# Attention followed by two MLP layers: where the two halves of an attention output are added, and where the gpsimd queue takes v_lo

## The reference

```python
# attention, B, H, S, D = 2, 8, 768, 64
q_bits = (einsum('bhsd,dk->bhsk', q, proj) > 0)          # 6 bits; k_bits alike
mask   = q_bucket[:, :, :, None] == k_bucket[:, :, None, :]
scores = where(mask, q @ k.T / 8, -1e9)
attn   = softmax(scores);  o = attn @ v                   # per head
# x = o as (1536, 512), then
h = x @ w_in;  g = s * relu(h)**2 + b;  y = g @ w_out     # d_ff = 2048
out = ((y @ w1) * (y @ w2)) @ w3 @ w_out2                 # d_ff = 1024
```

## Time and profile before

| | |
|---|---|
| median of 3 runs | 803.09 us (801.74 to 803.3) |
| the profiled execution | 801.51 us |
| its span | 799.7 us |
| PE busy | 765.9 us (96%) |
| DVE busy | 459.5 us (57%) |
| ACT busy | 369.8 us (46%) |
| POOL busy | 239.0 us (30%) |
| attention part | 0 to about 287 us |

### The profile page before, as it was taken

How to read it: one execution, slowest core, us unless ns; L and a number is a source line. 1 busy time by engine, 2 the same in 40 slices (tenths; PEclk the granted TensorE clock), 3 DMA queues, 4 the chain that set the end, 5 groups by cost and what they waited for, 6 DMA issues and landing times.

```text
span 799.7 us, 11232 instructions
## 1 busy us (share of the span) xinstructions
PE 765.9 (96%) x3680; PEld 626.1 (78%) x3680; DVE 459.5 (57%) x809; ACT 369.8 (46%) x686; POOL 239.0 (30%) x150
## 2 busy tenths in 40 slices
PE   3999999999989989999999999999999999999998
PEld 2787787877878778888888888888887888888886
DVE  4898998998979921276565665656575201210220
ACT  2887898888979942353223232222342211211211
POOL 3346564565655564663021120210012000000000
PEclk9999999999999999999999999999999999999999
DMA  6343333433353222233010110101010000001001
GB/s 148 78 118 74 75 92 83 110 75 84 80 135 84 66 88 86 100 105 106 2 52 1 53 53 0 52 0 53 1 52 1 1 32 21 1 14 39 0 0 52
DMA packets 17680, 45.37 MB, mean 57 GB/s; under 512 B 4946, under 2 KB 6994, under 8 KB 17650
## 3 DMA queue, kind: packets, MB, share of 16 engines
q1 hardware_dynamic: 17650, 44.99, 20.4%
HBM read 37.75 MB, written 3.19 MB: 51 GB/s over the span
## 4 chain that ended last, share of the span: by engine, by line
PE 72%; POOL 9%; DMA 6%; ACT 5%; issue 3%; DVE 3%; SPq 1%; POOLq 0%; ACTq 0%
PE psum L987 54%; PE psum L1074 8%; DMA r_sb<-r_rows 4%; PE psum L941 3%; ACT prob L525 3%; PE psum L928 3%; POOL x_raw L389 2%; POOL raw L364 2%; POOL km L374 1%; PE psum L917 1%; ACT pt_hi L541 1%; PE psum L911 1%; POOL both_hi L369 1%; POOL vs L379 1%; DVE x_lo L864 1%
## 5 line engine op out<-in xcount | busy, mean ns | idle before, releaser
L760 DVE TENSOR_TENSOR pt_lo<-psum,pt_hi 128x384 fp32r<-128x384 f32 x192 | 97.8, 550 | 19.5 <-ACT pt_hi L541 18.1
L525 ACT ACTIVATE prob<-psum,exp_at 128x768 f32<-128x768 f32 x96 | 96.4, 1005 | 10.3 <-DVE exp_at L753 10.2
L541 ACT ACTIVATE pt_hi<-psum 128x384 fp32r<-128x384 f32 x192 | 84.2, 494 | 27.9 <-PE psum L928 26.7
L746 DVE TENSOR_REDUCE top<-psum 128x1 f32<-128x768 f32 x96 | 90.9, 946 | 4.2 <-PE psum L917 4.0
L633 ACT ACTIVATE relu<-psum 128x512 f32<-128x512 f32 x48 | 28.6, 597 | 137.2 <-PE psum L987 137.2
L987 PE MATMUL psum<-x_hi,w_b 128*128 128x512 f32 (+1 forms) x288 | 90.6, 396 | 0.0
L987 PE MATMUL psum<-x_hi,w_c 128*128 128x512 f32 (+1 forms) x288 | 90.5, 396 | 0.0
L928 PE MATMUL psum<-ident,prob 128*128 128x128 f32 x576 | 83.4, 280 | 4.4 <-DVE pt_lo L760 4.1
L887 DVE TENSOR_TENSOR ab<-psum,a_sb 128x512 f32<-128x512 f32 x24 | 16.6, 692 | 121.3 <-ACT a_sb L683 121.3
L841 DVE SCALAR_TENSOR_TENSOR relu<-psum,relu 128x512 f32<-128x512 f32 x48 | 33.1, 689 | 87.9 <-ACT relu L633 82.8
L403 POOL TENSOR_TENSOR w_b<-stage,w_b 128x1024 fp32r<-128x1024 f32 x18 | 43.7, 2427 | 126.5 <-ACT w_b L552 125.8
(11 more groups left out here) (91 smaller groups left out, 1481.5 us busy)
## 6 DMA issues: line engine op xcount, KB each, us to landing
raw<-in_qk SPq DMA_DIRECT2D x30, 384.0 KB, 5.2
stage<-in_w_out SPq DMA_DIRECT2D x12, 512.0 KB, 3.3
stage<-in_w3t SPq DMA_DIRECT2D x8, 512.0 KB, 3.8
stage<-in_w_in SPq DMA_DIRECT2D x8, 512.0 KB, 3.2
stage<-in_w SPq DMA_DIRECT2D x8, 512.0 KB, 3.2
raw_v<-in_v SPq DMA_DIRECT2D x16, 192.0 KB, 2.8
qm<-both_hi SPq DMA_DIRECT2D x16, 192.0 KB, 2.7
r_sb<-r_rows SPq DMA_DIRECT2D x16, 192.0 KB, 5.4
```

Of the source, the lines that this page charges most:

```text
L525: act.activation(prob[:, t % 3], score[t % 2], ACT.Exp, bias=exp_at[:, t % 2, 1:2], scale=exp_at[:, t % 2, 0:1], accum_out=rsum[:, (t // 6 ...
L541: act.activation(pt_hi[:, u % 2, 3 * part:3 * part + 3, (t % 3) * P:(t % 3 + 1) * P], turned[part].rearrange("p (j q) -> p j q", j=3), ACT ...
L746: dve.tensor_reduce(top[:, t % 2, 1:2], score[t % 2], AX.X, ALU.max, negate=True).then_inc(top_done, 1)
L760: dve.tensor_tensor(pt_lo[at], turned[part].rearrange("p (j q) -> p j q", j=3), pt_hi[at].bitcast(F32), ALU.subtract).then_inc(pt_lo_done, 1)
```

## The change

ACT copies both halves out of PSUM: the one that changes rows into `o_part`, which now has two buffers, and the other into `o_sum`. Both count `o_part_done`, and PE may overwrite bank 6 after both. POOL adds them, in place in `o_sum`, directly before the product in `x_of`; DVE's `o_add` is gone. ACT's copies wait for the product of the unit four before (`x_done`) instead of the DVE's add. Since that count is not positive in pair 1, ACT's loop starts at pair 2 and pair 1 is written out. On POOL both v_lo of a pair come ahead of the x_of of the same stretch, and in the last two pairs the weight remainders change places with x_of. The scratch area for dynamic DMAs is set to 1024 bytes; the kernel has no such DMA.

```diff
-            o_part = sb("o_part", [P, HALF], F32, a)
+            o_part = sb("o_part", [P, 2, HALF], F32, a)
...
             def x_of(u, unit, pr):
+                rows = slice(0, HD) if unit < 2 else slice(HD, P)
+                pool.wait_ge(o_part_done, 2 * u + 2)
+                pool.tensor_tensor(o_sum[rows, unit % 2], o_sum[rows, unit % 2], o_part[rows, unit % 2],
+                                   ALU.add).then_inc(o_sum_done, 1)
                 pool.wait_ge(o_sum_done, u + 1)
...
                 if not first:
+                    v_lo(2 * pr, 0)
+                    pool.wait_ge(v_lo_done, 2 * pr + 1)
                     x_of(4 * pr - 2, 2, pr - 1)
                     pool.wait_ge(x_done, 4 * pr - 1)
+                if before_last:
+                    w_out2_low(0)
                 if not last:
                     scale_q(pr + 1, 1)
                     pool.wait_ge(q_scaled, 2 * pr + 4)
                 if not first:
-                    v_lo(2 * pr, 0)
-                    pool.wait_ge(v_lo_done, 2 * pr + 1)
-                    if before_last:
-                        w_out2_low(0)
-                    if last:
-                        w_out2_low(2)
                     x_of(4 * pr - 1, 3, pr - 1)
                     pool.wait_ge(x_done, 4 * pr)
                 if last:
+                    w_out2_low(2)
                     w_out2_low(3)
...
+                v_lo(2 * pr + 1, 1)
+                pool.wait_ge(v_lo_done, 2 * pr + 2)
                 x_of(4 * pr, 0, pr)
                 pool.wait_ge(x_done, 4 * pr + 1)
-                v_lo(2 * pr + 1, 1)
-                pool.wait_ge(v_lo_done, 2 * pr + 2)
                 if before_last:
                     w_out2_low(1)
-                if last:
-                    w_low(W3, high(w_b, 0), low(w_b, 0), 0)
-                    pool.wait_ge(w_lo_done, W3 + 1)
                 if not (last or before_last):
                     scale_q(pr + 2, 0)
                     pool.wait_ge(q_scaled, 2 * pr + 5)
                 x_of(4 * pr + 1, 1, pr)
                 pool.wait_ge(x_done, 4 * pr + 2)
+                if last:
+                    w_low(W3, high(w_b, 0), low(w_b, 0), 0)
+                    pool.wait_ge(w_lo_done, W3 + 1)
...
-                after(act, o_sum_done, u)
-                act.activation(o_part[dst], o_ps[src], ACT.Copy).then_inc(o_part_done, 1)
+                after(act, x_done, u - 3)
+                act.activation(o_part[dst, unit % 2], o_ps[src], ACT.Copy).then_inc(o_part_done, 1)
+                act.activation(o_sum[dst, unit % 2], o_ps[dst], ACT.Copy).then_inc(o_part_done, 1)
...
-            with act.Fori(1, PAIRS - 2) as pr:
+            pair(1)
+            with act.Fori(2, PAIRS - 2) as pr:
...
-            def o_add(u, unit):
-                dve.wait_ge(o_part_done, u + 1)
-                after(dve, x_done, u - 3)
-                rows = rows_of(unit)
-                dve.tensor_tensor(o_sum[rows, unit % 2], psum[rows, 6, 0:HALF], o_part[rows],
-                                  ALU.add).then_inc(o_sum_done, 1)
...
-                    if t % 3 == 0 and not (first and t < 6):
-                        o_add(u - 2, t // 3 + 2)
...
-            for k in range(2):
-                o_add(2 * HEADS - 2 + k, 2 + k)
...
-                    after(pe, o_sum_done, u)
+                    after(pe, o_part_done, 2 * u)
...
-    nc = bacc.Bacc("TRN2", target_bir_lowering=False, num_devices=1)
+    nc = bacc.Bacc("TRN2", target_bir_lowering=False, num_devices=1, dynamic_dma_scratch_size=1024)
```

More of the change, by code:

```diff
@@ L382, in x_of @@
             def x_of(u, unit, pr):
+                rows = slice(0, HD) if unit < 2 else slice(HD, P)
+                pool.wait_ge(o_part_done, 2 * u + 2)
+                pool.tensor_tensor(o_sum[rows, unit % 2], o_sum[rows, unit % 2], o_part[rows, unit % 2],
+                                   ALU.add).then_inc(o_sum_done, 1)
                 pool.wait_ge(o_sum_done, u + 1)
                 pool.wait_ge(r_in[unit // 2], 16 * (pr + 1))
-                rows = slice(0, HD) if unit < 2 else slice(HD, P)
                 at = slice((unit % 2) * HALF, (unit % 2 + 1) * HALF)
@@ L772, in inverse_sums @@
                 dve.reciprocal(rinv[:, par, :], rsum_e[:, par, :]).then_inc(rinv_done, 1)
-            def rows_of(unit):
-                return slice(0, HD) if unit % 4 < 2 else slice(HD, P)
-            def o_add(u, unit):
-                dve.wait_ge(o_part_done, u + 1)
-                after(dve, x_done, u - 3)
-                rows = rows_of(unit)
-                dve.tensor_tensor(o_sum[rows, unit % 2], psum[rows, 6, 0:HALF], o_part[rows],
-                                  ALU.add).then_inc(o_sum_done, 1)
             k_lo(0)
@@ L797, in pair @@
                     h, k = 2 * pr + t // 6, t // 6
-                    u = 4 * pr + t // 3
                     ahead = not (last and t > 8)
-                    if t % 3 == 0 and not (first and t < 6):
-                        o_add(u - 2, t // 3 + 2)
                     pt_low(n, t, 0)
```

## The result

| | before | after |
|---|---|---|
| median, 7 executions each, same chip | 802.40 us | 807.29 us (806.45 to 809.06) |
| ratio | | 1.0067, 95% interval 1.0052 to 1.0082 |
| the profiled execution | 801.51 us | 808.31 us |
| its span | 799.7 us | 806.6 us |
| PE busy | 765.9 us | 772.0 us |

The change makes the kernel slower, by 4.9 us of 802.4 between medians. The profiled executions lie 6.8 apart, because that of before is 0.9 under its median and that of after 1.0 over its own. The forecast was 806.0, within 800.3 to 809.5.

The account below looks back on a forecast made before the run. The prediction took a loop through POOL and the DMA queue as the attention stage's bound, then ACT near its end. Terms +0.9 - 0.9 + 1.8 + 0.8 + 0.3 = +2.9 on the median 803.09 gave 806.0 us, range 800.3 to 809.5.

Parts of the forecast that it names:

- the ring: Attention-stage loop through POOL, SyncE's queue and DMA; claimed to set the pace, 33.11 us for a pair of heads.
- K: End of the odd head's k_lo, POOL's last instruction of a pair; the next product was predicted 7.3 us later.
- pair 0: First pair: v_lo and the add now precede the first product, which starts 0.94 us late; +0.9 us.
- five periods: Looped pairs of the attention stage: shorter POOL work in the first half outweighs a later product; -0.17 each, -0.9 us.
- pair 6: Pair before last, straight code: ACT is full, v_high comes 0.4 late and POOL's chain delays PE's dots; +1.8 us.
- pair 7: Last pair: ACT has no idle time, three more copies cost 1.2, partly offset by hand-over and wait; +0.8 us.
- behind it: After the last pair: POOL's remaining work delays the next weight remainder about 1.1, with 0.8 of cover; +0.3 us.
- in the other half I take the cover as sufficient: Second half of each looped period: DMA time assumed to hide v_lo and add; otherwise 0.94 us more a period.
- third rival: POOL becomes the bound outright, PE's clock falls, or the second half's cover is missing (+4.7): 808 to 811 us, chance 0.15.
- odd lag: From the odd head's k_lo to the next product in the loop: predicted 7.3 us instead of 7.0, +0.3.
- The wait was the bound: Faster rival: v_lo first gives PE back 7.6 us of attention-stage stalls; 800.5 us, in full 797.5; chance 0.22.
- PE's clock falls: Part of the third rival: idle time before the dots lowers PE's clock and delays v_high, +2 us; shared chance 0.15.

Follow-up runs that it names:

- e1: Kernel before with only POOL's new order in every pair, weight remainders of the last two pairs included, DVE still adding: 793.94 us, ratio 0.9885.
- e2: Changed kernel with POOL's old order, weight remainders included; ACT copies both halves and POOL adds: 817.37 us, ratio 1.0173.
- e9: Changed kernel with only unit 0's add moved ahead of x_low and v_lo, in the even half: 805.34 us, ratio 1.002.
- e10: Changed kernel with only unit 2's add moved ahead of v_lo, in the odd half: 807.54 us, ratio 1.0047.
- e3: Changed kernel with the adds of units 0 and 2 moved ahead of v_lo, into POOL's wait for v_high: 800.99 us, ratio 0.9975.
- e7: Kernel before with only the two side edits, ACT's pair 1 written out and the 1024-byte DMA scratch area: 804.51 us, ratio 1.0003.
- e5: Changed kernel without POOL's 32 adds; ACT's two copies and the new order stay: 799.69 us, ratio 0.9952.
- e12: Kernel before with only the two v_lo of a pair moved ahead of their products; weight remainders stay, DVE adds: 793.53 us, ratio 0.9848.
- e4: Changed kernel with its order and both ACT copies, but DVE instead of POOL adds the halves, from SBUF: 804.72 us, ratio 1.0017.

## Why the prediction was right, and where it was off

**The direction and its reason hold.** The prediction said that the ring through POOL, not PE's visible stall, sets the period, that the stall would move to the dots (L899, now L886), and that ACT has no room in the last pair. The last two are in the profile; for the first speak e1 and e2, where POOL's order alone moves the period, and against its being the whole of it e9 and e10. Its price for the add, 0.99 us, is 1.009 in 32 rows, and its start of the product after K, K + 7.3, is 7.37 in the period shown and 7.43 in the mean. By the Trainium skill ("GPSIMD Engine Reference", section "Engine selection") adds belong on VectorE, POOL being about twice as slow; the trace agrees roughly, 1009 ns against 553, 1.8 times.

**Term by term**, from the two profiled executions (sum +6.9 in the span, against +2.9 predicted):

| term | predicted | measured | how |
|---|---|---|---|
| pair 0 | +0.9 | +1.31 | K 55.42 against 54.11 |
| five periods | -0.9 | +1.57 | K 55.42 to 222.56, against 54.11 to 219.68 |
| pair 6 | +1.8 | +2.20 | dots 260.25 against 255.17, less the 2.88 above |
| pair 7 | +0.8 | +0.95 | last value product +6.03, less 5.08 |
| behind it | +0.3 | +0.87 | 6.90 - 6.03 |

That the time came out within 1.3 us of 806.0 is in part luck. The change costs 4.9 us between medians and 6.9 in the profiles, where 2.9 was predicted, and every term is larger than predicted; 0.7 of the 2.0 is given back because the kernel before took 802.40 in the seven executions and not 803.09. Larger effects, which the sum doesn't price by themselves, also cancel in it, as shown below.

**The step that failed is in the term of the five periods: "in the other half I take the cover as sufficient".** The lag after the even k_lo grew by 0.65 in the mean (0.93 in the period shown), where the prediction put nothing. I had checked the first half against its 7.00 us and not the second against its 6.50. The second half has the same chain as the first: v_high ends 4.92 after k_lo in both (127.37 - 122.45; in the second half ACT's v_high starts at 143.50 and takes 0.53, so 144.03 - 139.11), and v_lo, add and their waits bring this to 7.4. The 6.50 and the sum for the odd half stood in the prediction, and so did the price of its failure, 0.94 a period: this is the missing cover that it lists with its third rival, at a chance of 0.15 for all of them together. The other parts of the period came out as walked or better: odd lag +0.43 (predicted +0.3), odd stretch -0.58 (-0.54), even stretch -0.18 (+0.07). At full clock the loop costs 0.47 a period where a gain of 0.17 was predicted, and this difference of 0.64 is about what the even lag grew.

That the adds behind v_lo cost this is shown by e3: with two of them out of the lags, these are back at 6.96 and 6.81, the period at 32.47, and the time at 800.99. That the even half by itself decides is not: e9 brings the even lag back to 6.77, and the period falls by 0.13 only, because the odd lag grows to 7.86. The prediction adds four parts of the period as if each could change by itself; e9 and e10 show that they can't.

How large the term is depends on which execution of the kernel before stands beside it. The profiled one holds one fall of the clock in the loop, which costs it about 1.0 of the five periods, and e7 two; against e7 the loop of the changed kernel looks free. At full clock it costs 0.47 a period, 2.3 us if taken five times, and the fall that the changed kernel no longer has gives about 1.0 back. The prediction has no term for this. The seven executions of the changed kernel all have a mean granted clock of 0.998, the 71 of the kernel before in the experiments 0.989 to 0.998: the 8 at 0.989 take 805.5 us in the mean, the 11 at 0.996 or more 801.9. So part of what separates two executions of the kernel before goes with the clock.

**ACT's copies were costed at nothing in the loop.** There the prediction charged them only in pairs 0, 6 and 7. e5 against e1 gives 799.69 - 793.94 = 5.8 us, 0.92 a period of it, with no add on POOL and none on DVE. The sum doesn't show it, and neither does it show e1's gain: the walk exchanged v_lo for the add, -1.15 for +1.16. That is right on POOL and says nothing of what each is worth alone. The order alone is worth 9.1 us. The books of the change, in medians: -9.1 for the order, +5.8 for ACT's copies, +7.6 for POOL's adds (807.29 - 799.69), together +4.2 against the 803.05 of that chip. By the ratios, which take out the chip, it is -9.2, +5.4 and +9.2 (0.9885, 0.9952 and 1.0067 of 802.4), together +5.4. So the adds cost 8 to 9 us and the copies 5 to 6, with an uncertainty, from the intervals, of some 2 us for the adds and 3 for the copies; the 9 of the order hold the falls of the clock that the kernel before has in the loop and e1 has not.

**The second copy** starts 0.51 after the first, not 0.40 (289.65 and 290.16): two pt_hi copies overlap more than these do. In pair 0 v_high starts at 43.67 instead of 43.36, and that is 0.31 of the 0.4 missed there; that the copies make it late is argued, not shown.

**The rivals.** "The wait was the bound" did not happen in the change, but it was argued from the wrong wait. It looked at PE's 7.6 us of stalls; what v_lo first gives is POOL's stretch, shorter by 1.37 and 0.94 us a pair, and e12 turns that into 1.7 a period. "PE's clock falls" had the wrong sign in the loop: the kernel before is at half clock in 67 to 68, and the changed kernel, which no longer stops for v_lo, is at full. Its window of that microsecond:

```profile
67.00:68.00 1.00, 0.97 (x7) 0.65 (x6) 0.90 (x2) 1.00 (x3) 0.92 (x2) 1.00 0.18 45
```

It does fall in pair 6 of both kernels (before near 231 to 234 us, after near 235 to 237).

**What stays open.** Why one add ahead gives next to nothing in the loop: in e9 and e10 what one lag loses the other gains back, through a later v_high, so PE and ACT seem to keep a pace of about 33.3 us per pair as long as one half is late. e5 has a floor of 32.3 with the copies in. No run separates what sets either, nor how much of a period with a fall of the clock is the stop and how much the slower clock.

## What to carry to other kernels

When an instruction is put ahead of another whose transfer is awaited, check the cover in every half of the period by the same sum; in e9 and e10 one short cover was enough to keep the period at 33.3. Compare loops over periods at the same granted clock before reading a difference under 1%. Split a change that moves an order and an engine at once: here the order alone took 9.1 us off and the engines put 13.4 back. An add that depends on nothing new belongs in the wait ahead of the instruction that waits, not behind it (e3, 6.3 us for the same work), in every half at once.

## What the runs showed of the hardware

- A DVE add of 64x384 with both inputs in SBUF took 0.55 us alone and 0.82 to 1.69 when it started while a POOL instruction was running, always ending 0.40 to 0.42 after that one (e4, 15 of 32). DVE's adds with one operand in PSUM took 0.54 to 0.56 in all 32, though 17 of them started beside a running POOL instruction, as here in the kernel before:

```profile
129.32 1.47 POOL L364 TENSOR_TENSOR raw<-raw,scale_col 128x768 f32<-128x768 f32 x1 [0.17 <-POOL x_raw L389]
...
129.68 0.56 DVE L782 TENSOR_TENSOR o_sum<-psum,o_part 64x384 f32<-64x384 f32 x1
```

By the Trainium skill ("SBUF — State Buffer", section "SBUF: two separate sides") a DVE instruction with two SBUF inputs and a GpSimd instruction that reads SBUF exclude each other for their whole length, and e4 agrees: at 132.10 POOL had 0.67 us to go, and the add took 0.53 longer.
- POOL's add with two 64x384 inputs took 1009 ns, no more than the v_lo subtraction of 128x384 (1006 ns): between 64 and 128 partitions it made no difference, the columns did. Nor at 768 columns (1838 ns for q_lo of 64x768, 1841 for x_low of 128x768).
- PE's granted clock fell to 0.50 of full after stops of 1.76 (before, at 65.39), 2.04 and 1.68 us (e7, at 66.19 and 100.27), and not after 1.79 (before, at 197.79) nor in the loop after four of 1.85 to 2.25 (e2). So the 1.76 and 1.57 that the prediction compares don't separate the two cases: the length of the stop alone doesn't tell. A period with such a fall took 0.9 to 1.4 us more than the others of its loop.
